# Second MLP of a fused attention and double-MLP kernel: second products grouped six by six, one sum moved on VectorE

## What is computed

```python
x = attention(q, k, v)                  # 4 x 8 heads, 576 keys, window 128, head size 64
x = reshape(x, (2304, 512))
x = square(maximum(x @ w_in, 0)) @ w_out       # first MLP:  512 -> 2048 -> 512
h = x @ w_in2                                  # second MLP: 512 -> 2048 -> 512
return (h * cos(h)) @ w_out2
```

## Time and profile before

| | |
|---|---|
| median of three runs | 858.27 us |
| the profiled execution | 858.33 us |
| its span, first to last instruction | 856.3 us |
| outside the span | 2.0 us |
| TensorE matmul busy | 845.1 us, 99% of the span |
| VectorE busy | 650.5 us, 76% |
| ScalarE busy | 524.9 us, 61% |
| mean granted TensorE clock | 1.000 (the 2.4 GHz level) |

### The profile page before, as it was taken

One profiled execution on the slowest core, in us unless ns is written; L12 is line 12 of the kernel. 1 busy time (PEld: TensorE's weight loads), 2 busy tenths in 40 slices (PEclk: granted clock), 3 DMA queues, 4 the chain that ended last, 5 costly groups with the idle time before them and its releaser, 6 DMA issues.

```text
span 856.3 us, 16170 instructions
## 1 busy us (share of the span) xinstructions
PE 845.1 (99%) x5846; PEld 766.4 (89%) x5846; DVE 650.5 (76%) x1455; ACT 524.9 (61%) x1145; POOL 79.4 (9%) x174
## 2 busy tenths in 40 slices
PE   7999999999999999999999999999999999999997
PEld 5888999999999999999999988889898998888896
DVE  6999979787687676696776777777877777767664
ACT  7999544342353333344333887777788777777774
POOL 7678600000000000000000000000000000000000
PEclk9999999999999999999999999999999999999999
DMA  7775716647588778779768555556565655664522
GB/s 240 229 247 179 283 57 257 215 161 257 204 294 310 245 276 315 254 243 321 284 242 296 183 197 185 162 195 197 197 227 192 197 178 179 221 236 161 194 74 74
DMA packets 72046, 185.34 MB, mean 216 GB/s; under 512 B 7200, under 2 KB 19488, under 8 KB 69920
## 3 DMA queue, kind: packets, MB, share of 16 engines
q1 hardware_dynamic: 71104, 183.23, 63.0%
q10 hardware_dynamic: 864, 1.08, 0.4%
HBM read 141.82 MB, written 42.47 MB: 215 GB/s over the span
## 4 chain that ended last, share of the span: by engine, by line
PE 95%; DVE 3%; ACT 1%; issue 1%; POOL 0%; DVEq 0%
PE psum L695 40%; PE psum L729 23%; PE psum L734 15%; PE psum L736 8%; PE psum L633 4%; PE psum L591 3%; PE psum L536 2%; DVE probs L1101 1%; PE psum L545 0%; DVE g_lo L1282 0%; ACT probs L823 0%; PE psum L553 0%; POOL probs L510 0%; DVE comb L1191 0%; DVE hidden_sum L1228 0%
## 5 line engine op out<-in xcount | busy, mean ns | idle before, releaser
L695 PE MATMUL psum<-xt_hi,comb 128*128 128x384 f32 x1344 | 394.4, 335 | 0.2
L695 PEld LDWEIGHTS psum<-xt_hi,comb 128*128 128x128 f32 x1344 | 248.0, 188 | 14.4 <-DVE hidden_sum L1228 0.4
L729 PE MATMUL psum<-wout,g_hi 128*128 128x512 f32 x576 | 179.2, 392 | 0.4 <-DVE g_lo L1282 0.4
L734 PE MATMUL psum<-g_hi,wout 128*128 128x512 f32 x384 | 148.9, 391 | 0.0
L1282 DVE TENSOR_TENSOR g_lo<-work,g_hi 128x384 fp32r<-128x384 f32 x192 | 102.5, 553 | 58.0 <-ACT g_hi L924 56.4
L924 ACT ACTIVATE g_hi<-work 128x384 fp32r<-128x384 f32 x192 | 97.4, 518 | 79.6 <-DVE work L1277 41.0
L695 PE MATMUL psum<-x_lo,comb 128*128 128x384 f32 x384 | 129.1, 336 | 0.0
L729 PEld LDWEIGHTS psum<-wout,g_hi 128*128 128x128 f32 x576 | 105.8, 188 | 13.2 <-issue 0.8
L729 PE MATMUL psum<-wout,g_lo 128*128 128x512 f32 x288 | 114.2, 397 | 0.0
L736 PE MATMUL psum<-g_hi,wout 128*128 128x256 f32 x384 | 107.5, 280 | 0.0
L695 PE MATMUL psum<-xt_lo,comb 128*128 128x384 f32 x288 | 96.6, 335 | 0.0
(11 more groups left out here) (94 smaller groups left out, 1282.9 us busy)
## 6 DMA issues: line engine op xcount, KB each, us to landing
comb<-comb SPq DMA_DIRECT2D x80, 768.0 KB, 5.0
wout<-wout SPq DMA_DIRECT2D x48, 512.0 KB, 4.9
comb<-comb SPq DMA_DIRECT2D x8, 1792.0 KB, 6.8
comb<-kept SPq DMA_DIRECT2D x8, 1792.0 KB, 6.9
wout_raw<-w_out SPq DMA_DIRECT2D x48, 256.0 KB, 6.0
comb<-comb SPq DMA_DIRECT2D x40, 256.0 KB, 3.1
v_raw<-v SPq DMA_DIRECT2D x16, 512.0 KB, 3.5
raw<-w_in SPq DMA_DIRECT2D x32, 256.0 KB, 7.1
```

The costliest lines, as they stand in the source:

```text
L695: last = pe.matmul(psum[:, H_BANK + i % 2, 0:NH], wi, mi[:, k, :], start=first, stop=True, skip_group_check=True)
L729: last = pe.matmul(psum[:, Y_BANK + c, :], g[:, r, tok], w, start=start and m == 0, stop=True, skip_group_check=True)
L734: pe.matmul(psum[:, Y_BANK + c, :], wi[:, w], g[:, r, 0:512], start=start and m == 0, stop=True, skip_group_check=True)
```

## The change

Two edits. In steps 26 to 32, 34 to 40 and 42 to 47 (20 steps: the second MLP without its first two steps and without the turn steps) the twelve pieces of a step no longer stand 2, 1, 2, 1, 2, 2, 2 behind the seven first products, but six behind product 2 (the third; the old strip) and six behind product 6 (the seventh; the new strip). Products 0, 1, 2 then follow each other directly, and so do 3, 4, 5, 6. Step 24 keeps 1, 1, 1, 1, 1, 1, 2.

On VectorE, in all steps of the second MLP with j other than 1, part_c_sum (after product 3) moves behind turn_high, turn_low and moving_sum, to stand right ahead of c22_sum (after product 4).

```diff
@@ pieces_after @@
-                return ((2, 1, 2, 1, 2, 2, 2) if (old if i < 4 else new) else (1, 1, 1, 1, 1, 1, 2))[i]
+                return ((0, 0, 6, 0, 0, 0, 6) if old else (1, 1, 1, 1, 1, 1, 2))[i]
@@ vector engine, second_step @@
                 if n < ALL:
-                    part_c_sum(n)
+                    if j == 1:
+                        part_c_sum(n)
                     turn_high(n, 0)
                     turn_low(n, 0)
                     if T_AT[j] and j != 1 and t + 1 < 2 * SUPERS:
                         moving_sum(t + 1, T_AT[j])
+                    if j != 1:
+                        part_c_sum(n)
                     c22_sum(n)
```

## The result

The changed kernel takes 859.66 us, the median of 22 runs, against 858.31 of the kernel before in the same comparison: a ratio of 1.0016, with a 95% interval of 1.001 to 1.0022. That is 1.35 us slower and 1.3 us above the forecast of 858.4. It lies inside the 0.2% that I had called no change, but the interval lies clear of 1: the change is a small loss, not nothing.

The account below looks back on a forecast made before the run. It took the pace of TensorE's matmuls as the bound, with no TensorE wait to remove in steps 25 to 47. 858.33 - 3.1 + 3.7 - 0.57 = 858.4 us; own range 857.6 to 859.4, whole range 857.2 to 861.5.

Parts of the forecast that it names:

- the pace: TensorE, 20 steps: longer runs of one kind save 0.155 us a step, -3.1 us; lower bound nothing.
- Stalls behind the turn steps: Steps 26, 34, 42: product 2 waits 1.25 us for ScalarE's copy of part_a, +3.7 us (3.6 to 3.9).
- The sums in time in ordinary steps: Ordinary steps: part_c_sum and c22_sum release products 5 and 6 in time, 0 us, at most 2.4 in 20 steps.
- The margin of 0.04 us: Products 5 and 6: release allows the second matmul at s + 1.34, needed at s + 1.38.
- The two parts as I wrote them: Per step: pieces 8.34 to 8.24 us, saving 0.10; first products 7.355 to 7.29, saving given as 0.06.
- two at 1.045 behind six pieces: Each of the 20 steps: the two first products behind six pieces take 1.045 us each.
- The tail: Strip 95's wait for lo_g of quarter 2 of step 47 goes: -0.57 us, at worst 0.
- The moved sum: VectorE: left in place, part_c_sum would push turn_low and moving_sum between it and c22_sum, costing a stall.
- The pace doesn't depend on the order: Rival: the 4.12 us of six pieces belong to the tail, so no pace saving; 861.5 us, chance 0.10.
- The two sums are late in each step: Rival: 0.06 us lost at product 5 and at product 6 in 20 steps, +2.4; 860.8 us, chance 0.20.
- The stalls don't come: Rival: no stalls behind the turn steps, because ScalarE's queue is lighter there; 854.7 us, chance 0.10.
- the order doesn't arrive as written: Rival: on TensorE the first of six pieces waits on its g strip; no price, chance 0.02.

Follow-up runs that it names:

- Experiment one: Changed kernel, but steps 26, 34 and 42 keep the old pieces 2, 1, 2, 1, 2, 2, 2: 856.25 us, ratio to before 0.9978.
- seven: Changed kernel with pieces 0, 2, 4, 0, 2, 0, 4 in steps 26, 34, 42 and the weights wait moved from product 5 to 4: 855.88 us, ratio 0.9976.
- experiment four: Changed kernel with TensorE's wait for the last group of loaded weights moved from product 5 to product 4: 859.56 us, ratio to before 1.0012.
- experiment six: Changed kernel with pieces 0, 2, 4, 0, 2, 0, 4 in all 20 steps: 857.7 us, ratio to before 0.9994.
- experiment eight: Changed kernel with the old pieces 2, 1, 2, 1, 2, 2, 2 in steps 26, 34, 42 and also 47: 856.82 us in one profiled execution.
- experiment three: Changed kernel with the old pieces 2, 1, 2, 1, 2, 2, 2 back, so only part_c_sum is moved: 858.24 us, ratio to before 0.9994.
- experiment five: Kernel before with pieces 2, 2, 2, 0, 2, 2, 2 in the same 20 steps, part_c_sum not moved: 857.07 us, ratio 0.9988.

## Why the prediction was right, and where it was off

The mechanism held, and so did the wide range (857.2 to 861.5) with its larger chance on the slower side. The forecast itself said no change, +0.1 us, and the kernel is 1.35 slower. The range of the sum, 857.6 to 859.4, was missed by 0.3 us. Nearly all of the difference lies in one term, the pace. The steps one by one:

**Stalls behind the turn steps, +3.7.** Right in place, number and size: three, of 1.25 us (622.37 against 621.12). Experiment one removes them and gains 3.4 us, with the pace of three steps given back; seven fills them.

**The sums in time in ordinary steps, 0, at most 2.4.** Right as to VectorE: before part_c_sum it had 0.95 us in hand without moving_sum and 0.07 to 0.08 with it; in steps 26 and 34 it came 0.01 to 0.02 late, without a listed wait. The margin of 0.04 us behind it was too fine. Product 5 takes 0.01 to 0.027 more in nearly every step, and experiment four shows that its second wait is the cause. Product 6 takes 0.02 to 0.03 more in seven steps. In the twenty steps that is 0.4 and 0.2 us, 0.6 together.

**The pace, -3.1.** This is the term that was mis-sized. Per step 0.155 was expected and 0.087 measured (15.687 less 15.600), -1.7 us in 20 steps. (The two parts as I wrote them, 0.10 and 0.065, give 0.165; the difference to the 0.155 of the sum is small against the miss.) The pieces kept their part: 4.12 us for six, as in the tail. The products didn't: the step that failed is "two at 1.045 behind six pieces". I carried the price of a product behind two pieces over to one behind six. Measured are 1.066 behind six, four (experiment six) and three pieces, 1.061 behind one and 1.044 behind two. The trace of before had it in sight, just ahead of the earlier trace rows, in turn step 33:

```profile
609.46 0.33 PE L695 MATMUL psum<-xt_hi,comb 128*128 128x384 f32 x1
```

This is the first matmul of product 2, behind three pieces. Product 3 starts 0.18 behind 610.35, at 610.53: 1.066 for the product. Two of these a step are 2 x 0.021 = 0.042, and product 5 adds up to 0.026, together the missing 0.07. The turn steps 33 and 41, whose product 0 now stands behind six pieces instead of two, pay the same 0.02 each.

**The tail, -0.57.** Right in kind: the wait is gone, and experiment eight brings it back by undoing step 47. It was worth a little more than its length. In the kernel before, this row follows 843.13 by four pieces:

```profile
845.97 0.62 PE L729 MATMUL psum<-wout,g_hi 128*128 128x512 f32 x2
```

These four take 2.84 us, where four pieces deep in a run take 2.72: behind the wait the slower pace of the start of a run came once more. From product 0 of step 47 to the last matmul it is 28.40 us before and 27.61 after, 0.79 less, of which the step itself is 0.09. So the tail gave 0.7.

**The moved sum.** That it is needed was right, and its worth measured: 871.5 - 859.7 = 11.8 us. Alone it does nothing (experiment three).

The sum with the measured terms: 858.31 - 1.7 + 3.7 + 0.04 - 0.7 = 859.65, against 859.66. The traces agree: from product 0 of step 24 to the last matmul it is 389.01 us before and 390.37 after, 1.36 more; the medians differ by 1.35.

**The rivals.** "The pace doesn't depend on the order" falls with experiment five, where only the pieces were moved, and with 4.12 us for six pieces; but only a good half of the pace term came. "The two sums are late in each step" is true in part: product 5 in each step, product 6 in seven, at a quarter of its price (0.6 of 2.4 us). "The stalls don't come" is refuted by the waits. The last, that the order doesn't arrive as written, too: the timeline shows six pieces in a run.

What stays open: why a product is slower behind one, three, four or six pieces than behind two. The runs show the numbers and no mechanism.

## What to carry to other kernels

Where TensorE never waits, an order of its work is priced twice: by the pace of each kind behind each other kind, read from starts over whole steps, and by the shortest distance between a result and the product that needs it. Check that distance in the worst step, not in the usual one: here three steps behind a block change, where ScalarE was 1.45 us later than elsewhere, ate what twenty others and the tail had gained. If only those few steps fail, give them an order of their own.

## What the runs showed of the hardware that I had not expected

- The same three matmuls over 512 columns take 0.70 us in the first piece of a run, 0.69 in the second and third and 0.68 from the fourth on (step 36 and the tail of the changed kernel). Behind a wait inside a run it starts anew: 0.77, 0.69, 0.70, 0.68 in the tail of the kernel before.
- A release can cost without being seen as a wait. By the count from the earlier trace rows part_c_sum released product 5 some 0.04 us before it was needed, and the product still took 0.01 to 0.027 us more. In the ordinary steps the weight load of product 5 started 0.005 to 0.007 us behind the last matmul of product 4, and one that nothing holds up starts 0.002 to 0.003 behind: a load late by a few nanoseconds costs the product more than that. With one wait less in front of it product 5 was back at 1.04, but product 6 took 1.045 to 1.07 instead.
- The attention part differs between executions by more than this change is worth, although the kernels are equal there. Step 24 came 2.5 us later in the trace of experiment four than in that of the changed kernel (the last matmul of its product 0 at 464.84 against 462.37). These are rows of two stretches in each, experiment four first (stretch; its length, TensorE busy and matmuls, granted clock, share of the DMA engines, GB/s):

```profile
10.00:17.20 7.20, 4.27 (x57) 1.00 0.91 314
17.20:20.60 3.40, 3.40 (x39) 0.50 0.55 200
```

```profile
10.00:17.20 7.20, 4.62 (x73) 1.00 0.89 299
17.20:20.60 3.40, 3.34 (x76) 1.00 0.66 217
```

For 3.4 us TensorE was granted half its clock (0.50, the 1.2 GHz level) and did 39 matmuls instead of 76. Before that it had been busy 4.27 of 7.2 us at full clock. About 1.0 us of the 2.5 was there before the clock fell (the 100th matmul started at 12.98 against 11.97), so the clock isn't the whole cause. What set off either part the runs don't show. Hence the medians of many runs, and the comparison of stretches within a trace.
